# Order of the score products, places of the first twelve units' stages, and the engine that scales the front parts' pooled probabilities

## Reference

```python
q_d, k_d, v_d = (a.reshape(B, H, 144, 4, D).mean(axis=3) for a in (q, k, v))
out_d = sm_attn(q_d, k_d, v_d)                       # softmax attention over 144 pooled positions
out_up = np.repeat(out_d, 4, axis=2)
mask = np.abs(pos[:, None] - pos[None, :]) < 4
scores = np.where(mask, scale * q @ k.T, -1e9)       # local: a band of 7 keys
attn = softmax(scores)                               # divided by its sum + 1e-9
x = out_up + attn @ v                                # (2304, 512)
h = np.maximum(np.maximum(x @ w1, x @ w2), x @ w3)   # 768 wide
y = h @ w_out                                        # 512
g = np.maximum(0.01 * (y @ w_in), y @ w_in)          # 2048 wide
out = g @ w2_out                                     # (2304, 512)
```

## Time and profile before

| | us |
|---|---|
| median of 3 runs (797.06 to 797.6) | 797.56 |
| the profiled execution, its own time | 798.22 |
| its span, first to last instruction | 796.4 |
| TensorE busy | 775.4 (97%) |
| VectorE busy | 411.0 (52%) |
| ScalarE busy | 273.8 (34%) |
| GpSimd busy | 125.1 (16%) |
| mean granted clock of TensorE | 0.989 |

### The profile page before, as it was taken

How to read it: one execution, slowest core, us unless ns; L and a number is a source line. 1 busy time by engine, 2 the same in 40 slices (tenths; PEclk the granted TensorE clock), 3 DMA queues, 4 the chain that set the end, 5 groups by cost and what they waited for, 6 DMA issues and landing times.

```text
span 796.4 us, 13494 instructions
## 1 busy us (share of the span) xinstructions
PE 775.4 (97%) x5470; PEld 706.6 (89%) x5470; DVE 411.0 (52%) x743; ACT 273.8 (34%) x662; POOL 125.1 (16%) x168
## 2 busy tenths in 40 slices
PE   8779899999999999999999999999999999999998
PEld 7767889989999999999998888899898899998986
DVE  6666677866555433423245566665344457434333
ACT  4355343443333222222144444353222234222222
POOL 4566312111111000011023334310000000000000
PEclk9889999999999999999999999999999999999999
DMA  8362233323121003003045735446424325422312
GB/s 296 116 218 67 85 114 98 110 81 100 51 86 46 1 23 129 0 34 110 21 139 208 266 146 181 203 141 244 143 93 164 113 93 180 175 94 93 128 58 79
DMA packets 29342, 94.19 MB, mean 118 GB/s; under 512 B 2784, under 2 KB 15072, under 8 KB 26208
## 3 DMA queue, kind: packets, MB, share of 16 engines
q1 hardware_dynamic: 29280, 93.33, 33.6%
HBM read 69.21 MB, written 24.12 MB: 117 GB/s over the span
## 4 chain that ended last, share of the span: by engine, by line
PE 93%; DVE 4%; issue 2%; ACT 1%; DVEq 0%; ACTq 0%
PE mlp_ps L866 13%; PE mlp_ps L868 12%; PE mlp_ps L867 12%; PE mlp_ps L953 7%; PE mlp_ps L951 7%; PE mlp_ps L952 7%; PE att_ps L972 6%; PE att_ps L974 6%; PE att_ps L973 6%; PE mlp_ps L972 3%; PE mlp_ps L974 3%; PE mlp_ps L973 3%; PE att_ps L855 2%; PE att_ps L768 1%; PE att_ps L816 1%
## 5 line engine op out<-in xcount | busy, mean ns | idle before, releaser
L866 PE MATMUL mlp_ps<-x_hi,wa_lo 128*128 128x432 f32 (+1 forms) x432 | 151.6, 351 | 0.0
L868 PE MATMUL mlp_ps<-x_hi,wa_hi 128*128 128x432 f32 (+1 forms) x432 | 146.7, 340 | 0.0
L867 PE MATMUL mlp_ps<-x_lo,wa_hi 128*128 128x432 f32 (+1 forms) x432 | 146.7, 340 | 0.0
L866 PEld LDWEIGHTS mlp_ps<-x_hi,wa_lo 128*128 128x128 f32 x432 | 82.7, 191 | 5.6 <-issue 2.3
L867 PEld LDWEIGHTS mlp_ps<-x_lo,wa_hi 128*128 128x128 f32 x432 | 82.7, 191 | 2.1
L868 PEld LDWEIGHTS mlp_ps<-x_hi,wa_hi 128*128 128x128 f32 x432 | 82.5, 191 | 2.2
L1162 ACT ACTIVATE h_hi<-wa_raw 128x384 fp32r<-128x384 f32 x72 | 37.5, 523 | 102.1 <-DVE wa_raw L1417 101.1
L1346 DVE TENSOR_TENSOR h_raw<-mlp_ps,half_max 128x432 f32<-128x432 f32 (+1 forms) x36 | 20.0, 555 | 74.9 <-PE mlp_ps L868 74.7
L1415 DVE TENSOR_TENSOR wa_raw<-mlp_ps,h_raw 128x384 f32<-128x384 f32 x24 | 13.4, 558 | 86.2 <-PE mlp_ps L953 54.3
L1429 DVE TENSOR_TENSOR h_lo<-wa_raw,h_hi 128x384 fp32r<-128x384 f32 x72 | 44.9, 631 | 22.3 <-ACT h_hi L1162 20.3
L972 PE MATMUL att_ps<-wa_hi,h_lo 128*128 128x512 f32 x132 | 52.7, 399 | 0.7 <-DVE h_lo L1429 0.7
(11 more groups left out here) (162 smaller groups left out, 1740.4 us busy)
## 6 DMA issues: line engine op xcount, KB each, us to landing
u_even<-u_scratch SPq DMA_DIRECT2D x8, 1792.0 KB, 7.3
u_odd<-u_scratch SPq DMA_DIRECT2D x8, 1664.0 KB, 6.4
kq_in<-in_kq SPq DMA_DIRECT2D x14, 576.0 KB, 4.0
u_scratch<-u_even SPq DMA_DIRECT2D x4, 1792.0 KB, 8.4
u_scratch<-u_odd SPq DMA_DIRECT2D x4, 1664.0 KB, 6.6
v_rows<-in_v_sum SPq DMA_DIRECT2D x16, 288.0 KB
wa_raw<-in_w SPq DMA_DIRECT2D x6, 768.0 KB, 5.6
v_win<-in_v_band SPq DMA_DIRECT2D x12, 384.0 KB, 3.5
```

What stands on the lines that cost most here:

```text
L866: nc.tensor.matmul(ps, wlo, xhi, start=(n == 0), stop=False)
L867: nc.tensor.matmul(ps, whi, xlo, start=False, stop=False)
L868: last = nc.tensor.matmul(ps, whi, xhi, start=False, stop=(n == len(pairs) - 1))
```

## The change

Three things are edited. (1) `STAGE_JOBS` and `scores(u)`: for every unit but 0, TensorE makes the pooled scores first and the local ones after them; VectorE takes the pooled maximum first and only then waits for the local scores. (2) `first_phase()`: `S4`, `E4` and `D5` move ahead of `Ma3`, `D4` ahead of `V3`, `X0,3` ahead of `S4`; `LQ4` to ahead of `M0`; the stages of units 4 to 11 get new places, `V` of the later ones a little later ones; `D` comes 1.5 instead of 1.3 ahead of `S`; `X1,3` goes from group 18 to group 20. (3) On front parts `N u` no longer scales `prob_g` on VectorE: ScalarE does it with two activations (`normalise(u)`), a wait for the reciprocal ahead of them. VectorE's next reciprocal waits until ScalarE has read the one before.

The diff, cut to its core:

```diff
-        ("Ma", 0), ("V", 3), ("LV", 5), ("WL", 4), ("WL", 5), ("Ma", 1), ("Ma", 2), ("Ma", 3), ("X", 0, 3))
+        ("Ma", 0), ("D", 4), ("V", 3), ("LV", 5), ("WL", 4), ("WL", 5), ("Ma", 1), ("Ma", 2), ("X", 0, 3), ("S", 4),
+        ("E", 4), ("D", 5), ("Ma", 3))
...
-    put(0.3, ("D", 4), ("S", 4), ("E", 4))
-    put(1.2, ("D", 5))
-    put(1.5, ("LQ", 4))
-    put(2.2, ("S", 5), ("E", 5))
-    put(2.5, ("LQ", 5))
+    put(0, ("LQ", 4))
+    put(1.2, ("S", 5), ("E", 5))
+    put(1.5, ("LQ", 5))
...
-    plan = {4: (1.5, 4, 5, 6), 5: (5.2, 7.7, 8.7, 9.7), 6: (8.9, 11.4, 12.4, 13.6), 7: (12.6, 15, 16, 17),
-            8: (15.3, 19.3, 20.3, 22), 9: (20.8, 24.3, 25.3, 27), 10: (25.8, 29.3, 30.3, 32), 11: (30.8, 34.3, 35.3, 37),
+    plan = {4: (2, 5.2, 6.2, 7.7), 5: (6.4, 9, 10, 11.6), 6: (10.2, 12.8, 13.8, 15.6), 7: (13.9, 16.4, 18.3, 19.6),
+            8: (15.2, 20.4, 21.4, 23.4), 9: (21.7, 24.7, 25.7, 27.7), 10: (26.2, 29.5, 30.5, 32.5), 11: (31.2, 34.5, 35.5, 37.5),
...
-            put(s_at - 1.3, ("D", u + 2))
+            put(s_at - 1.5, ("D", u + 2))
...
-        put(NM * (c - 1) + HG + 1, *(("X", c, kk) for kk in range(KM)))
+        for kk in range(KM):
+            put(NM * (c - 1) + HG + (2.3 if c == 1 and kk == KM - 1 else 1), ("X", c, kk))
...
-STAGE_JOBS = {"S": ("sl0", "sl1", "sg0", "sg1"), "T": ("dt0", "dt1", "lt0", "lt1"), "V": ("up", "av0", "av1")}
+STAGE_JOBS = {"S": ("sg0", "sg1", "sl0", "sl1"), "T": ("dt0", "dt1", "lt0", "lt1"), "V": ("up", "av0", "av1")}
...
+            def scores(u):
+                if u == 0:
+                    local_scores(u)
+                    pooled_scores(u)
+                else:
+                    pooled_scores(u)
+                    local_scores(u)
...
-                pe.wait_ge(probs_ready, 2 * u + 1)
+                if part == FRONT:
+                    pe.wait_ge(prob_g_ready, u + 1)
+                else:
+                    pe.wait_ge(probs_ready, normalised(u) - 1)
...
+            def normalise(u):
+
+                nq = PART_GROUPS[FRONT][0][1]
+                act.wait_ge(inv_ready, u + 1)
+                for i in range(2):
+                    last = nc.scalar.activation(prob_g[:nq, u % 2, i, :], prob_g[:nq, u % 2, i, :], ACT.Copy,
+                                                scale=row_inv[:nq, SLOTS + i:SLOTS + i + 1])
+                last.then_inc(prob_g_ready, 1)
...
+                if 0 < u <= PAIRS:
+
+                    dve.wait_ge(prob_g_ready, u)
+                nc.vector.reciprocal(row_inv[:, :], sums).then_inc(inv_ready, 1)
+                dve.wait_ge(inv_ready, u + 1)
+                if part != FRONT:
+                    nc.vector.tensor_tensor(glob, glob, row_inv[:nq, SLOTS:SLOTS + 2 * ng].unsqueeze(2).to_broadcast([nq, 2 * ng, SD]),
+                                            ALU.mult).then_inc(probs_ready, 1)
```

More of the change, by code:

```diff
@@ L206, with stage_jobs @@
 ZERO_BANK = 3
-STAGE_JOBS = {"S": ("sl0", "sl1", "sg0", "sg1"), "T": ("dt0", "dt1", "lt0", "lt1"), "V": ("up", "av0", "av1")}
+STAGE_JOBS = {"S": ("sg0", "sg1", "sl0", "sl1"), "T": ("dt0", "dt1", "lt0", "lt1"), "V": ("up", "av0", "av1")}
+def stage_jobs(item):
+    kinds = STAGE_JOBS.get(item[0], ())
+    return kinds[2:] + kinds[:2] if item[:2] == ("S", 0) else kinds
 def bank_of(kind, u):
@@ L223 @@
 for _item in FIRST:
-    for _kind in STAGE_JOBS.get(_item[0], ()):
+    for _kind in stage_jobs(_item):
         if _kind in ("dt1", "lt1") and UNITS[_item[1]][1] != WHOLE:
@@ L404, in build @@
         exp_done = sem("exp_done")
+        prob_g_ready = sem("prob_g_ready")
         probT_evac = sem("probT_evac")
@@ L424, in build @@
         shifted = sem("shifted")
+        inv_ready = sem("inv_ready")
         probs_ready = sem("probs_ready")
@@ L484, in build, with normalised @@
         w_hi, w_lo, w_raw = (wa_hi, wo_hi), (wa_lo, wo_lo), (wa_raw, wo_raw)
+        def normalised(u):
+            return u + 1 if u < PAIRS else PAIRS + 2 * (u - PAIRS + 1)
         def x2_part(n):
@@ L538, in load_kq @@
                 if p >= PAIRS:
-                    sp.wait_ge(att_done, JOB["sg1", p if p < PAIRS + 2 else p + 2] + 1)
+                    sp.wait_ge(att_done, JOB["sl1", p if p < PAIRS + 2 else p + 2] + 1)
                 sp.dma_start(kq_of(p), kq[divmod(p, PAIRS)]).then_inc(kq_loaded[p % PAIRS], 16)
@@ L752, in begin, with local_scores @@
                     pe.wait_ge(s, count)
-            def scores(u):
+            def local_scores(u):
                 p, part = UNITS[u]
@@ L781, in scores, with pooled_scores @@
                                          start=False, stop=True).then_inc(att_done, 1)
+            def pooled_scores(u):
+                p, part = UNITS[u]
                 pe.wait_ge(sums_ready, u + 1)
@@ L811, in transposes @@
                         last.then_inc(att_done, 1)
-                pe.wait_ge(probs_ready, 2 * u + 2)
+                pe.wait_ge(probs_ready, normalised(u))
                 for i, (s0, s1) in enumerate(LT[part]):
@@ L1117, in _ @@
                     exps(item[1])
+                elif item[0] == "N" and UNITS[item[1]][1] == FRONT:
+                    normalise(item[1])
                 elif item[0] == "T":
@@ L1245, in shifts @@
                     dve.wait_ge(att_done, JOB[f"lt{len(LT[UNITS[u - 2][1]]) - 1}", u - 2] + 1)
-                dve.wait_ge(att_done, JOB["sl1", u] + 1)
                 scores = att_ps[:, 0:2, 0:ns * TQ].rearrange("p h (s w) -> p h s w", w=TQ)
                 by_head = local.rearrange("p (h s) w -> p h s w", h=2)
[L1249 to L1253, removed]
                 dve.wait_ge(att_done, JOB["sg1", u] + 1)
@@ L1260, in shifts @@
                 nc.vector.tensor_reduce(max_g.rearrange("p (h n) -> p h n", h=2), src, AX.X, ALU.max).then_inc(max_ready, 1)
+                dve.wait_ge(att_done, JOB["sl1", u] + 1)
                 if part != FRONT:
+                    nc.vector.tensor_tensor(by_head, scores,
+                                            mask[:, :, :].rearrange("p (h s) w -> p h s w", h=2)[:, :, m0:m1, :], ALU.add
+                                            ).then_inc(masked, 1)
+                    scores = by_head
                     dve.wait_ge(masked, u + 1 - PAIRS)
```

## The result

| | before | changed |
|---|---|---|
| median, us | 797.31 (795.79 to 797.6, 4 runs) | 786.41 (785.7 to 788.58, 4 runs) |
| ratio to before, 95% interval | | 0.9872 (0.9847 to 0.9896) |
| the profiled execution, own time / span | 798.22 / 796.4 | 785.7 / 783.9 |

The change saves 10.9 us, and the forecast of 786.1 was 0.3 off. The kernel before has one run more here than ahead of the prediction (795.79), so its median is 797.31 and no longer 797.56. The changed kernel was timed once more beside later experiments: 786.18 us (784.09 to 786.78), ratio 0.9853 (0.9839 to 0.9866).

What follows compares the result with a forecast made beforehand. TensorE was taken as the bound wherever attention stages don't hold it up. Recovered 14.5 less 5.15 kept or new gives 9.3, plus 2.2 in the front: 11.5 us, from 797.56 to 786.1; range 782.5 to 791.5.

Steps and rivals of the forecast that it cites:

- The 3.6 us wait: Unit 4's transposes (T4): they start with no wait, so 3.59 us and 1.97 of lower clock behind it go.
- Group 6 and GpSimd: At M6 TensorE waits for weight block 2 from GpSimd, ready at A+6.3 against A+5.7: 0.6 us charged.
- T7: Unit 7's local transposes wait for V6's `combine`, behind N8: 1.6 to 2.9 us, 2.6 charged, plus 1.55 for the clock.
- V8 and T9: V8's `combine` ends just when T9 wants the bank: 0.4 us charged.
- The order of scores: Maximum about 0.74 us earlier, V a group later for units 8 to 10: L855's 4.5 us and 1.58 idle go.
- The rival that the order does nothing: VectorE comes to the maximum late anyhow; places and scaling alone count, 790.0 us; no chance of its own given.
- The front: Up to V3: 1.6 us earlier if the clock still falls at about 29.5, 2.9 if not; 2.2 taken.
- S1's wait for D1: In the front, pooled-first order makes S1 wait for D1, which ends at 9.77; no size given.
- The sum: Whole kernel: 14.5 recovered less 5.15 kept or new is 9.3 from 41.5 us on, plus 2.2 in front: 11.5.
- GpSimd as the bound: Rival at M6, M9, M12 and M15: tiles at 1.0 us instead of 0.604, 800.4 us, decisive from about 0.92; chance 0.04.

Runs made afterwards that it cites:

- experiment 3: Changed kernel with the old places in `first_phase()`, new order of scores and ScalarE scaling kept: 795.93 us, ratio 0.9989.
- experiment 7: Changed kernel with weight block 2 split behind V3 instead of behind M0 and E5: 784.7 us, ratio 0.9862.
- experiment 12: The changed kernel itself timed again, nothing edited: 786.18 us, ratio 0.9853.
- experiment 5: Changed kernel with N8 placed behind V6 (15.7 instead of 15.2): 787.39 us, ratio 0.988.
- experiment 6: Changed kernel with N8 placed behind the low half that group 18 needs (18.1 instead of 15.2): 784.68 us, ratio 0.9857.
- experiment 1: Changed kernel with the old order of scores (local first), new places and ScalarE scaling kept: 786.48 us, ratio 0.9865.
- 4: Changed kernel with the old order of scores and VectorE scaling, so the new places alone: 786.44 us, ratio 0.9877.
- experiment 2: Changed kernel with the pooled probabilities of front parts scaled on VectorE again: 787.22 us, ratio 0.9878.
- experiment 10: Changed kernel with weight block 2 early, N8 late, group sums early in the front, old order of scores and VectorE scaling: 787.09 us, ratio 0.9874.

## Why the prediction was right, step by step

*The 3.6 us wait* was right in mechanism and size. T4 starts at 44.55 with no wait, the clock is 1.00 behind it, and experiment 3 brings back the wait (2.87) and a lower clock (47 to 51 us) with the old places.

*Group 6 and GpSimd* was right in mechanism and too small: 0.6 charged, 1.21 measured, and experiment 7 shows that it is GpSimd. Counted from the end of M0 (39.4), GpSimd's last tile ended after 6.7 us where 6.3 was charged, because ScalarE's half came 0.3 later; TensorE was there after 5.9 instead of 5.7; and it went on only at 46.52, 0.4 us behind GpSimd's end, for which the prediction had no term.

*T7* was right: 2.6 charged within 1.6 to 2.9, 2.22 measured, released by `combine`, with the clock down for 3.4 us behind it in the first profile (and not in the second one of experiment 12). The reason was taken too narrowly. The prediction blamed N8 ahead of V6, and experiment 5 shows that to put V6 ahead only hands the wait on. Experiment 6 shows that there is room behind group 18.

*V8 and T9*, 0.4 us charged, did not come. Unit 5's local transposes waited 0.51 us instead, which the prediction did not charge.

*The order of scores* is the step that failed in its reason. The prediction gave two grounds for the end of L855's waits, the maximum 0.74 us earlier and V a group later, and the places alone do it: with the old order the waits stay away (experiments 1 and 4), and with the old places those of units 5 and 7 come back, unit 7's in part under another name (experiment 3). The prediction gave V a group more for units 8 to 10 only; its own list has it for 5 and 6 too. And it had no term for what freed unit 7: N8 no longer stands ahead of S9's maximum. The rival that the order does nothing was right on that point and wrong in its price: it expected 790.0 from places and scaling alone, and the places alone gave 786.44. Its price came mostly from the waits of units 6 and 7 staying. They stay only where VectorE comes to the maximum late, and with the new places it doesn't.

*The front* gave 3.1 us in the profiled execution (V3 starts at 33.33; it was 36.44), in which the clock stayed up, where 2.9 was forecast for that case and 2.2 charged. S1's wait for D1 was 1.35 and S3's 0.90, which the prediction named without a size. In two of the four executions the mean clock was 0.993, and five profiles of this front put V3 at 32.5 to 35.5. The 1.19 us saved by the scaling was not visible as time (experiment 2). In part the collision only moved on by one instruction: the changed kernel's L1328, which took that place beside GpSimd, ran 0.82 us in the mean where L1288 had taken 0.55.

*The sum*: 9.3 + 2.2 = 11.5 charged, and 9.4 + 3.1 = 12.5 between the two profiled executions, cut at V3; 10.9 between the medians. The 9.3 came out within 0.1, but partly because errors cancel: 0.6 too little at group 6 and 0.5 not charged at unit 5, against 0.4 too much at T7 and 0.4 at T9. That the forecast met the median within 0.3 us is luck as well, since the front alone differs by 3 us between executions.

*GpSimd as the bound* didn't come: 28 tiles beside a busier VectorE took 17.32 us, 0.62 each against the 0.92 from which it would have decided.

## What to carry to other kernels

When all engines walk one list, first ask which engine is full in which stretch. Moving its work out of the stretch removes the wait (experiment 6), swapping two items within it hands the wait on (experiment 5), and reordering work on an engine that waits anyhow pays nothing (experiment 1). An item moved away also frees whatever stood behind it, so follow the engine's list to the next maximum or copy that a bank waits for. Undo each part of a bundle by itself and do each alone before you credit it: here one of three parts carried nearly all of it. When a part of the kernel starts at another time in each execution, compare what stands behind it by itself: the medians hide experiment 6, the stretch behind V3 shows it. When a wait is put down to an engine that ended long before, look for the semaphore that the page doesn't name, and test it by moving that work.

## What the runs showed of the hardware

**GpSimd and VectorE.** One VectorE step with both inputs in SBUF (72 x 576) took 0.76 us alone and 1.50 or 2.43 us beside GpSimd. A VectorE step on 14 columns took 4.50 us, over eight GpSimd instructions in a row and not just one (experiment 10). The Trainium skill ("SBUF — State Buffer", Who interferes with whom) says of the port that both share that the loser is blocked for "the whole instruction" of the other. The step of 1.50 us agrees with that: it ended at 73.75, 0.6 us behind the GpSimd instruction that ended at 73.13. The 2.43 and 4.50 us go beyond it, since they reach over the end of one GpSimd instruction and over further ones. GpSimd is held up too: its sum at 73.21 took 1.93 us beside two such VectorE steps, 0.72 alone. That it was the port is argued from the end times, not shown.

**The clock without long gaps.** When the fillers were gone, TensorE's granted clock fell to 0.50 twice between 10 and 35 us (mean from 8 to 35 us 0.68), though TensorE never stood still for more than 2.2 us at a time. It had worked 19.05 of the 27 us, against 23.37 with fillers at 1.00. The Trainium skill ("TensorE: Matmul & The Clock Gate") has a rule for each reading. Under "HAM oscillation" it is long gaps that lower the clock, and by that it would have stayed up; under "A second HAM failure mode: psum-queue depth-cycling" frequent short idles between groups of products lower it too, and the run agrees with that one. The price was 1.9 us by the ratios and 3.0 by the medians. Fillers are no full guard: in the profile of experiment 2 the clock fell in the front with them in place.
